# Up products in Strassen's form, down sums in SBUF, and attention with 64-row heads

## The reference

```python
# attention: q, k, v are (2, 8, 768, 64)
state = gamma * state + k_t (outer) v_t      # gamma = 1 - 2 ** (-5 - head)
y_t = (q_t @ state) / sqrt(64)
# x: y as (1536 tokens, 512)
xn = x / sqrt(mean(x * x) + 1e-6) * rms_g
x = (silu(xn @ w_gate) * (xn @ w_val)) @ w_out           # 512 -> 1536 -> 512
p = domain_probs / (domain_probs.sum(-1) + 1e-9)
out = sum over e of p[:, e] * (relu(x @ w1[e]) @ w2[e])  # 4 experts, 512 -> 1024 -> 512
```

## Time and profile before

| | us |
|---|---|
| median of 3 runs (lowest 908.95, highest 910.52) | 909.82 |
| span of the profiled execution | 908.6 |
| TensorE busy | 884.0 |
| DVE / GpSimd / ScalarE busy | 272.7 / 216.4 / 161.7 |
| first FFN matmul starts | 83.38 |
| last FFN matmul starts | 903.79 |

### The profile page before, as it was taken

How to read it: one execution, slowest core, us unless ns; L and a number is a source line. 1 busy time by engine, 2 the same in 40 slices (tenths; PEclk the granted TensorE clock), 3 DMA queues, 4 the chain that set the end, 5 groups by cost and what they waited for, 6 DMA issues and landing times.

```text
span 908.6 us, 10971 instructions
## 1 busy us (share of the span) xinstructions
PE 884.0 (97%) x4070; PEld 731.1 (80%) x4070; DVE 272.7 (30%) x378; ACT 161.7 (18%) x285; POOL 216.4 (24%) x130
## 2 busy tenths in 40 slices
PE   7878999999999999999999999999999999999998
PEld 6766788888788888888888888888888888888886
DVE  5789723232423233312121212121212121212122
ACT  3563511111112121211111111111111111111110
POOL 3855300026402015620006500016400036200000
PEclk9998999999999999999999999999999999999999
DMA  8960200002200001300002200003200013001011
GB/s 303 336 242 9 96 0 0 0 4 101 82 0 1 0 0 59 104 24 0 0 1 85 101 0 0 0 6 110 69 0 0 0 32 107 1 0 46 1 46 47
DMA packets 18503, 45.71 MB, mean 50 GB/s; under 512 B 1840, under 2 KB 7984, under 8 KB 18480
## 3 DMA queue, kind: packets, MB, share of 16 engines
q1 hardware_dynamic: 18480, 45.39, 14.8%
HBM read 42.24 MB, written 3.15 MB: 50 GB/s over the span
## 4 chain that ended last, share of the span: by engine, by line
PE 89%; DVE 5%; issue 2%; ACT 2%; DMA 1%; DVEq 0%; SPq 0%; ACTq 0%
PE bank L423 29%; PE bank L424 29%; PE bank L425 29%; DMA q_blocks<-qkv 1%; PE bank L349 1%; DVE guess_sq L669 1%; DVE xs L677 1%; DVE x_lo L663 1%; DVE sumsq L657 1%; DVE probs L635 0%; DVE rstd L672 0%; ACT L537 0%; DVE h_lo L737 0%; DVE state L649 0%; PE bank L387 0%
## 5 line engine op out<-in xcount | busy, mean ns | idle before, releaser
L423 PE MATMUL bank<-x_hi,ffn_weights 128*128 (+1 forms) x672 | 261.9, 390 | 0.0
L425 PE MATMUL bank<-x_lo,ffn_weights 128*128 (+1 forms) x672 | 261.4, 389 | 0.0
L424 PE MATMUL bank<-x_hi,ffn_weights 128*128 (+1 forms) x672 | 261.4, 389 | 0.0
L790 DVE SCALAR_TENSOR_TENSOR h_lo<-bank,h_hi 128x512 fp32r<-128x512 f32 x96 | 66.3, 691 | 363.1 <-ACT h_hi L613 362.7
L423 PE MATMUL bank<-ffn_weights,h_hi 128*128 128x512 f32 x384 | 149.5, 389 | 0.2 <-DVE h_lo L790 0.2
L424 PE MATMUL bank<-ffn_weights,h_lo 128*128 128x512 f32 x384 | 149.4, 389 | 0.0
L425 PE MATMUL bank<-ffn_weights,h_hi 128*128 128x512 f32 x384 | 149.4, 389 | 0.0
L423 PEld LDWEIGHTS bank<-x_hi,ffn_weights 128*128 128x128 f32 x672 | 126.2, 188 | 26.4 <-issue 0.2
L425 PEld LDWEIGHTS bank<-x_lo,ffn_weights 128*128 128x128 f32 x672 | 126.1, 188 | 26.3
L424 PEld LDWEIGHTS bank<-x_hi,ffn_weights 128*128 128x128 f32 x672 | 126.2, 188 | 26.2 <-issue 0.2
L613 ACT ACTIVATE h_hi<-bank 128x512 fp32r<-128x512 f32 x96 | 57.6, 600 | 456.2 <-PE bank L425 456.2
(11 more groups left out here) (57 smaller groups left out, 546.8 us busy)
## 6 DMA issues: line engine op xcount, KB each, us to landing
raw<-w SPq DMA_DIRECT2D x32, 512.0 KB, 3.3
raw<-w SPq DMA_DIRECT2D x12, 768.0 KB, 4.5
ring<-qkv SPq DMA_DIRECT2D x10, 768.0 KB, 8.5
...
ring<-qkv SPq DMA_DIRECT2D x2, 512.0 KB, 5.5
decay_mask<-t_decay_mask SPq DMA_DIRECT2D x1, 512.0 KB, 4.3
```

The lines of the kernel that those rows point to most:

```text
L423: pe.matmul(dst, w_hi, m_hi, start=first, stop=False)
L424: pe.matmul(dst, w_lo, m_hi, start=False, stop=False)
L425: return pe.matmul(dst, w_hi, m_lo, start=False, stop=last)
L790: nc.vector.scalar_tensor_tensor(out=h_lo[:, j % 2, :], in0=bank[j % 2][:, :], scalar=0.0, in1=h_hi[:, j % 2, :].bitcast(F32), op0=ALU.max ...
```

## The change

Tokens are now in four blocks of 384, two (a = 0, 1) in each half j of 768. A **unit** is one pair of column tiles for one half j: in the first FFN the gate and the value of tile f, in the second two neighbouring tiles. Its 2 x 2 x 2 product (two token blocks, two halves of the features, two column tiles) is done as seven products instead of eight, in Winograd's form. Each product has two feature tiles and three passes, 6 matmuls of 384 columns. S1 to S4 are sums of x, T1 to T4 sums of weights.

```diff
-                for r in range(PAIRS):
-                    mm = pe.matmul(bank[2 * (s % 2) + r // 2][:, 256 * (r % 2):256 * (r % 2) + 256],
-                                   ring[:, s, 0, P * r:P * r + P], q_blocks[:, s, r, :], start=True, stop=True)
+                for r in range(PAIRS):
+                    for a in range(2):
+                        rows, cols = slice(DH * a, DH * a + DH), slice(CH * r, CH * r + CH)
+                        mm = pe.matmul(bank[2 * (n % 2) + a][:, cols], ring[rows, n % 4, 0, cols],
+                                       ring[rows, n % 4, 1, cols], start=True, stop=True)
...
-                    for k in range(KT):
-                        c = slice(DM * part + P * k, DM * part + P * k + P)
-                        mm = three_passes(bank[2 * (j % 2) + part][:, :], W1[:, j, 0, c], W1[:, j, 1, c],
-                                          x_hi[:, g, k, :], x_lo[:, g, k, :], k == 0, k == KT - 1)
+                for kt in range(2):
+                    mm = three(bank[3 * s + b][:, 0:TB], w_hi[c % 2][:, WS[ws], kt, :], w_lo[c % 2][:, WS[ws], kt, :],
+                               x_hi[j][:, XS[xs], kt, :], x_lo[j][:, XS[xs], kt, :], first and kt == 0, kt == 1)
...
+                elif name == "M6":
+                    pe.wait_ge(u_copied, 3 * q + 1)
+                elif name == "M7":
+                    pe.wait_ge(u_copied, 3 * q + 2)
+                elif name == "M4":
+                    pe.wait_ge(u_copied, 3 * q + 3)
+                elif name == "M3":
+                    pe.wait_ge(c22_ready, q + 1)
...
+            def reload_w(c):
+                sp.wait_ge(up_done, NP * (last_unit(c - 2) + 1))
+                load_w(c)
...
+                product(q, f, j, k, "M1")
+                product(q, f, j, k, "M5")
+                some(0, 1)
+                product(q, f, j, k, "M6")
+                product(q, f, j, k, "M2")
+                some(1, 2)
+                product(q, f, j, k, "M7")
+                some(2, 4)
+                product(q, f, j, k, "M4")
+                product(q, f, j, k, "M3")
```

1433 lines of the change are left out of this document (837 added, 596 removed).

## The result

The changed kernel takes **939.96 us** (median of 4 runs, 937.84 to 945.03) where the kernel before takes 909.38 (4 runs, 908.55 to 910.52): 1.0346 times as long, 95% interval 1.0327 to 1.0366. The forecast was 897 with a range of 878 to 914: wrong in size and in sign.

The account below looks back on a forecast made before the run. TensorE, busy 97% of the span, was taken as the bound. Attention 83.0, matmuls 763.0, first join 24.4, later waits 3.3, 2.7, 6 and 9, end 4.6 gave 896.0; with 1.2 added, 897 us, range 878 to 914.

Parts of the forecast that it names:

- GpSimd beside DVE, costed at nothing in layer 1: Layer 1: DVE operations with two SBUF inputs can stretch beside GpSimd; new pieces at most 1.9 us, so no cost.
- w(2): Layer 1: TensorE waits 3.3 us for column tile 2's weights, loaded and split only once unit 2 is through.
- Five first tiles, 6 us: Five layer 1 units: first down tile waits for h of the unit just before, 1.2 us each, 6 together.
- Attention, 83.0: Attention before the FFN: first up product starts at 83.0 us, for 83.4 before; ScalarE's order decides its end.
- Scores overlap: Attention: two 64-row loads overlap, scores take 0.85 us a step, not 1.7; part of a rival at 879 us, chance 0.15.
- First join, 24.4 beyond its matmuls: First FFN units after attention, through the eight down tiles: waits for copies, sums and h cost 24.4 us beyond the matmuls.
- Second join, 9: Layer 1 to layer 2: tiles waiting for DVE, then copies and sums holding units 24 and 25, 9 us together.
- 2928 matmuls of 384 columns at 171.5 ns: Up products and layer 1 down tiles: 171.5 ns per matmul, the middle between 169.8 and 173.1.
- the fixed reading: 384-column matmuls: the 13.1 ns beyond array time is a fixed part, so one takes 173.1 ns.
- Units of layer 2, 15.4 us without a wait: Steady units of layer 2: TensorE takes 15.4 us each, with no idling.
- DVE's order in the steady units: Rival, steady units: c22's sum comes late in DVE's order, 0.5 us more in each of 56 units; 925 us, chance 0.09.
- weight load: Rival, 384-column matmuls: each waits for the end of a 0.19 us load, 49 us more; 946 us, chance 0.04.

Follow-up runs that it names:

- no_split: Changed kernel with later weights not loaded, summed or split (GpSimd's weight operations shrunk to one or 16 columns; output not the reference's): 914.62 us.
- w_pieces: Changed kernel with the lo parts of each weight tile made in another order, each piece with its own signal: 933.82 us.
- half_pieces: Changed kernel with GpSimd's lo parts of the weights made in pieces of 256 columns instead of 512: 926.62 us.
- att_order: Changed kernel with the third feature sum straight after the tenth attention output, and ScalarE's last outputs ahead of the hi parts of S1 to S4: 933.79 us.

## Why the prediction was wrong, point by point

- **GpSimd beside DVE, costed at nothing in layer 1**: the step that failed, and the largest. The working had the rule, from the earlier trace rows, and set it aside because the new pieces are at most 1.9 long and DVE has slack in a unit. Two things were missed. A pair of held operations pays once for each (1.61 and 1.61 for 0.55 and 0.56), and the slack of the unit's sum doesn't help an operation on which TensorE waits next; the forecast itself had h_lo with 1.2 us too little cover. Measured by no_split: 21.3 us in the rest of layer 1, about 15 of them holds, which stood at nothing, and about 5 the w(2) chain, which stood at 3.3. It isn't the only one: without this work the kernel takes 914.62, still slower than before and at the edge of the range, by the terms below that came out too small (384 columns 5.6, spacing 6.8, second join 5.9, attention 5.0).
- **Five first tiles, 6 us**: right by themselves. Without GpSimd they wait 0.97 each (I had 1.2); with it 14.9 together and two of them with 16 and 8 starts at the 1.2 GHz level behind.
- **w(2), 3.3**: by its own numbers it is 3.3 + 8.7 - 9.1 = 2.9. Measured 4.7 and some 1.6 in the starts at the lower clock behind it; w_pieces takes away 6.
- **Attention, 83.0**: measured 88.0. ScalarE's order was foreseen, step by step, and is there. Scores overlap, as the rival had it (16 passes in 1.16 us in seven of the twelve steps, 1.87 to 2.08 in the others), yet nothing came of it: DVE's normalisations took 5.22 and 7.51 us for four, and not 2.2; the first of the two held the last states, the other the lo parts of x. half_pieces gives 2.0 to 3.9 of the 5.0 back. The same cause again, though the orders of TensorE and ScalarE weigh more here: att_order starts the first product at 72.9.
- **First join, 24.4 beyond its matmuls**: measured 21.4 (44.0 - 22.6 at the price of the forecast). The waits came in the places and sizes named: M6 waited 3.02 for M1's copy, M7 3.38 for U2's, the first tile 3.71 for h.
- **Second join, 9**: 4.6 for the tiles at layer 1's end stood (their waits are 1.49, 0.55, 1.18, 1.23 and four short ones); behind them 10.4 for 4.4: 2.6 for c22, 2.2 for an out_acc sum, and 16 starts at the lower clock, which I had not reckoned there.
- **2928 matmuls of 384 columns at 171.5 ns**: 173.4, the fixed reading. Choosing the middle cost 5.6 us. The bounds held. The Trainium skill's 162.5 ns for it, by "TensorE: Matmul & The Clock Gate", section "Back-to-back issue gap", is shown by no run here.
- **512 columns at 226.4 in layer 2**: 230.6 on the mean there, and 384 at 175; 6.8 us together, a cost that no term had. By the spacing above it goes with the changes between 384 and 512 columns, which the kernel before doesn't have; the reason is open.
- **Units of layer 2, 15.4 us without a wait**: measured 15.6 and no idle time from 500 to 900. The rivals "DVE's order in the steady units" and "weight load" are false: no steady unit of layer 2 waits, and the distance is 173 to 175 with a load record of 0.19. (By 0.19 - 0.1715 the second would have cost 54 and not 49.)
- **The sign.** The saving in matmuls is real: 815.0 us before, 2928 x 0.1734 + 1152 x 0.2264 = 768.5 now, 46.5 less. But from the first product to the end of the last matmul the changed kernel takes 846.6, so 78.1 are not matmuls at that price, where it was 5.6 before (4.7 + 0.9). That is 26 more than nothing gained; attention adds 4.6 and the end takes 1.2 off: 29.4, the difference of the two spans. The forecast gave 45.4 for the 78.1. The 32.7 above it are 23.2 in the rest of layer 1 (18.0 of them GpSimd's, 21.3 for 3.3), 5.9 in the second join and 6.8 of layer 2's spacing, less 3.2 in the first join.

The Trainium skill, page "SBUF — State Buffer", section "Who interferes with whom", has a DVE instruction with two SBUF inputs and a GpSimd one that reads SBUF exclude each other for a whole instruction. This case agrees instruction by instruction: the two h_lo operations at 288 us end at 290.10 and 291.63, the two GpSimd instructions beside them at 289.69 and 291.22, and the pair takes 1.23 where GpSimd has nothing to do.
